# A retention, mixture-of-experts and MLP kernel on one core: a warm-up of 72 small matmuls, tiles amid the turns of attention, and loads in rows of 2 KB

## The reference

```python
# 1. retention: q, k, v are [2, 8, 576, 64]
scores = q @ k.T / 8;  Dmat[h] = gamma_h ** (i - j) for i >= j, else 0
x = ((scores * Dmat) @ v) laid out as [1152, 512]          # tokens x model
# 2. four experts, all used, weighted by p = probs / sum(probs)
out = sum_e p[:, e] * (relu(x @ w1[e]) @ w2[e])            # w1 512x1024, w2 1024x512
# 3. one MLP
h = out @ w_in;  g = h * tanh(softplus(h));  y = g @ w_out # 512x2048, 2048x512
```

## Time and profile before

| | before |
|---|---|
| median of 3 runs | 621.67 us |
| profiled execution, its own time | 622.52 us |
| its span | 620.7 us |
| PE busy / DVE / ACT / POOL | 98% / 43% / 38% / 45% |
| matmuls | 4016 |
| granted PE clock, mean | 0.989 of full |
| DMA | 50.47 MB, mean 81 GB/s |

### The profile page before, as it was taken

The page is one execution under the profiler, slowest core; times in us unless marked ns, Lnnn a source line. Parts: engine busy times, 40 slices in busy tenths (PEclk is TensorE's granted clock), DMA queues, the critical chain, the costliest instruction groups (busy, mean ns, idle before and its releaser), DMA issues.

```text
span 620.7 us, 9829 instructions
## 1 busy us (share of the span) xinstructions
PE 605.9 (98%) x4016; PEld 547.0 (88%) x4016; DVE 264.0 (43%) x361; ACT 234.7 (38%) x434; POOL 278.2 (45%) x230
## 2 busy tenths in 40 slices
PE   6799999999999999999999999999999999999997
PEld 4699799999999999999999999989989999989996
DVE  2467654423154434154534154535545432324334
ACT  2464433322323332223432123435455454334431
POOL 2658645535335544435552535532446553443300
PEclk9699999999999999999999999999999999999999
DMA  8963202332112331112322112321211232201002
GB/s 345 331 213 109 80 35 68 104 101 68 35 35 68 103 103 57 46 35 68 102 84 62 58 34 69 102 69 37 67 34 49 69 105 84 68 1 52 1 1 101
DMA packets 24923, 50.47 MB, mean 81 GB/s; under 512 B 2864, under 2 KB 2992, under 8 KB 24880
## 3 DMA queue, kind: packets, MB, share of 16 engines
q1 hardware_dynamic: 24736, 49.84, 25.1%
q10 hardware_dynamic: 144, 0.02, 0.0%
HBM read 47.49 MB, written 2.36 MB: 80 GB/s over the span
## 4 chain that ended last, share of the span: by engine, by line
PE 92%; DVE 2%; ACT 2%; issue 1%; DMA 1%; POOL 1%; SPq 0%
PE bank L494 30%; PE bank L496 29%; PE bank L495 29%; PE bank L442 1%; DMA loaded<-in_feats 1%; PE bank L470 1%; PE bank L612 1%; PE bank L474 1%; ACT xt L736 0%; ACT w_hi L368 0%; DVE acc_sb L888 0%; DVE acc_sb L892 0%; POOL w_lo L395 0%; DVE xs_a L962 0%; DVE xs_a L959 0%
## 5 line engine op out<-in xcount | busy, mean ns | idle before, releaser
L395 POOL TENSOR_TENSOR w_lo<-w_raw,w_hi 128x512 fp32r<-128x512 f32 x96 | 134.6, 1416 | 149.8 <-ACT w_hi L368 149.8
L494 PE MATMUL bank<-w_hi,h_hi 128*128 128x512 f32 x432 | 168.7, 391 | 0.0
L496 PE MATMUL bank<-w_hi,h_lo 128*128 128x512 f32 x432 | 168.3, 390 | 0.0
L495 PE MATMUL bank<-w_lo,h_hi 128*128 128x512 f32 x432 | 168.3, 390 | 0.0
L875 DVE TENSOR_TENSOR h_act<-part,bank 128x384 f32<-128x384 f32 x96 | 52.9, 551 | 169.9 <-PE bank L496 169.4
L390 POOL TENSOR_TENSOR ws<-ws_f,ws 128x1024 fp32r<-128x1024 f32 x24 | 57.6, 2401 | 145.1 <-ACT ws L364 145.1
L496 PEld LDWEIGHTS bank<-w_hi,h_lo 128*128 128x128 f32 x432 | 81.1, 188 | 16.9
L495 PEld LDWEIGHTS bank<-w_lo,h_hi 128*128 128x128 f32 x432 | 81.1, 188 | 12.3
L494 PEld LDWEIGHTS bank<-w_hi,h_hi 128*128 128x128 f32 x432 | 81.0, 188 | 12.1
L722 ACT ACTIVATE part<-bank 128x384 f32<-128x384 f32 x72 | 35.3, 491 | 138.6 <-PE bank L496 138.6
L842 DVE SCALAR_TENSOR_TENSOR h_lo<-h_act,h_hi 128x384 fp32r<-128x384 f32 x64 | 73.2, 1153 | 20.5 <-ACT h_hi L712 19.9
(11 more groups left out here) (88 smaller groups left out, 863.0 us busy)
## 6 DMA issues: line engine op xcount, KB each, us to landing
w_raw<-in_weights SPq DMA_DIRECT2D x144, 256.0 KB, 2.7
loaded<-in_toks SPq DMA_DIRECT2D x9, 512.0 KB, 7.0
loaded<-in_feats SPq DMA_DIRECT2D x8, 512.0 KB, 6.2
out<-acc_sb SPq DMA_DIRECT2D x6, 256.0 KB, 2.1
out<-acc_sb SPq DMA_DIRECT2D x1, 768.0 KB, 3.5
loaded<-in_first SPq DMA_DIRECT2D x1, 726.0 KB, 4.4
ident<-in_ident SPq DMA_DIRECT2D x1, 64.0 KB, 5.0
p_nat<-in_probs ACTq DMA_DIRECT2D x1, 18.0 KB, 5.1
```

The source lines that it names most:

```text
L395: pool.tensor_tensor(w_lo[layer][:, x], w_raw[:, r % RAW], w_hi[layer][:, x].bitcast(F32), ALU.subtract).then_inc(s_wl, 1)
L494: pe.matmul(out, w[0], x[0], start=first, stop=False, **more)
L495: pe.matmul(out, w[0], x[1], start=False, stop=False, **more)
L496: return pe.matmul(out, w[1], x[0], start=False, stop=last, **more)
```

## The change

- `WARM_START, WARM_NEXT = 7, 5` become `WARM = 72`: 72 zero matmuls of 64x64 weights by 64 columns ahead of the first scores, none behind them.
- Tiles 0, 1, 2, 4 and 5 move from behind `output(c)` to between `scores_and_state(c)` and `output(c)` of the same turn (`TILE_AMID`); 3, 6 and 7 stay behind (`TILE_AFTER`). ACT and DVE take up the tiles amid at the end of their turn.
- The weight jobs of turn 1 and some others move one turn later or join others; `rows(i)` is computed in turns 0 to 3 and not 0 and 4 to 7.
- Features and tokens lie in memory as two blocks of 2 KB rows each, not as one of 4 KB rows; the load has one more dimension, the bytes are the same.
- Behind the turns DVE makes the first two differences before it splits tile 7, and the last `first_lo` comes behind the third and the first `t_lo`; ACT does the two weight jobs before the four `t_hi`.

```diff
-TILES_IN = {3: (0,), 4: (1,), 5: (2, 3), 6: (4,), 7: (5, 6), 8: (7,)}
-JOBS_IN = {1: (("w1", 0, 0),), 2: (("w1", 0, 1), ("w1", 0, 2)), 3: (("w1", 0, 3),), 4: (("w1", 0, 4), ("w1", 0, 5)),
-           5: (("w1", 0, 6),), 6: (("w1", 0, 7), ("w2", 0, 0)), 7: (("w2", 0, 1), ("w2", 0, 2), ("s", 0, 0)),
-           8: (("w2", 0, 3), ("w2", 0, 4)), 9: (("w2", 0, 5),)}
+TILE_AMID = {3: 0, 4: 1, 5: 2, 6: 4, 7: 5}
+TILE_AFTER = {5: 3, 7: 6, 8: 7}
+JOBS_IN = {2: (("w1", 0, 0), ("w1", 0, 1)), 3: (("w1", 0, 2),), 4: (("w1", 0, 3), ("w1", 0, 4)),
+           5: (("w1", 0, 5), ("w1", 0, 6)), 6: (("w1", 0, 7), ("w2", 0, 0)),
+           7: (("w2", 0, 1), ("w2", 0, 2), ("s", 0, 0)), 8: (("w2", 0, 3), ("w2", 0, 4)), 9: (("w2", 0, 5),)}
-ROWS_IN = {4: 5, 5: 6, 6: 7, 7: 8}
+ROWS_IN = {0: (2, 3), 1: (4, 5), 2: (6,), 3: (7, 8)}
-WARM_START, WARM_NEXT = 7, 5
+WARM = 72
...
-                sp.dma_start(slots[:, c % SLOTS, 0:2], feats_in[c - 1]).then_inc(s_feats[c % SLOTS], 16)
+                sp.dma_start(slots[:, c % SLOTS, 0:2].rearrange("p w h c -> p w (h c)"), feats_in[c - 1].rearrange("w p k -> p w k"))\
+                  .then_inc(s_feats[c % SLOTS], 16)
...
-                    pe.matmul(banks[7][:, :], zeros[:, 0:P], zeros[:, :], start=True, stop=True)
+                    pe.matmul(banks[7][HALF[0], 0:CH], zeros[:, 0:CH], zeros[:, 0:CH], start=True, stop=True)
...
-            keep_warm(WARM_START)
+            keep_warm(WARM)
...
-            keep_warm(WARM_NEXT)
             for c in range(PLACES):
                 if has_state(c):
                     scores_and_state(c)
+                if c in TILE_AMID:
+                    early_tile(TILE_AMID[c])
                 output(c)
-                for t in TILES_IN.get(c, ()):
-                    s, i = divmod(t, ITEMS)
-                    plain_ready(s, i)
-                    plain_products(s, i, range(KT))
+                if c in TILE_AFTER:
+                    early_tile(TILE_AFTER[c])
...
+                if c in TILE_AMID:
+                    plain_hi(*divmod(TILE_AMID[c], ITEMS))
+            for job in IN_STAGE[1]:
+                job_hi(act, job)
             for n in range(4):
                 t_hi(0, n)
-            for job in IN_STAGE[1]:
-                job_hi(act, job)
...
-            first_lo(PLACES - 1)
+                if c in TILE_AMID:
+                    plain_lo(*divmod(TILE_AMID[c], ITEMS))
...
+            dve.wait_ge(s_xt, PLACES)
             dve.tensor_tensor(full[0], b12, b11, ALU.subtract).then_inc(s_tf, 1)
-            dve.tensor_tensor(full[2], b22, b12, ALU.subtract).then_inc(s_tf, 1)
             dve.wait_ge(s_tf, 1)
             dve.tensor_tensor(full[1], b22, full[0], ALU.subtract).then_inc(s_tf, 1)
-            dve.wait_ge(s_tf, 3)
+            plain_lo(*divmod(TILE_AFTER[PLACES - 1], ITEMS))
+            dve.tensor_tensor(full[2], b22, b12, ALU.subtract).then_inc(s_tf, 1)
+            t_lo(0, 0)
+            first_lo(PLACES - 1)
+            dve.wait_ge(s_tf, 2)
             dve.tensor_tensor(full[3], full[1], b21, ALU.subtract).then_inc(s_tf, 1)
-            dve.wait_ge(s_tf, 4)
-            for n in range(4):
+            for n in range(1, 4):
                 t_lo(0, n)
```

More of the change, by code:

```diff
@@ L402, in load_feats @@
             def load_feats(c):
-                sp.dma_start(slots[:, c % SLOTS, 0:2], feats_in[c - 1]).then_inc(s_feats[c % SLOTS], 16)
+                sp.dma_start(slots[:, c % SLOTS, 0:2].rearrange("p w h c -> p w (h c)"), feats_in[c - 1].rearrange("w p k -> p w k"))\
+                  .then_inc(s_feats[c % SLOTS], 16)
             def load_toks(c):
-                sp.dma_start(slots[:, c % SLOTS, 2:4], toks_in[c]).then_inc(s_toks[c % SLOTS], 16)
+                sp.dma_start(slots[:, c % SLOTS, 2:4].rearrange("p w h c -> p w (h c)"), toks_in[c].rearrange("w p k -> p w k"))\
+                  .then_inc(s_toks[c % SLOTS], 16)
             def load_weights(r):
@@ L522, in plain_products, with early_tile @@
                     mm.then_inc(s_l1, 1)
+            def early_tile(t):
+                s, i = divmod(t, ITEMS)
+                plain_ready(s, i)
+                plain_products(s, i, range(KT))
             def product(s, j):
@@ L734, in t_hi @@
                 i = T_ORDER[n]
-                act.wait_ge(s_tf, (9, 8, 6, 10)[n] if e else (3, 2, 1, 4)[n])
+                act.wait_ge(s_tf, (9, 8, 6, 10)[n] if e else (2, 3, 1, 4)[n])
                 act.activation(x_sum(i, 0), x_full(e, i), ACT.Copy).then_inc(s_th, 1)
@@ L740, in _ @@
                     first_hi(c - 1)
-                for t in TILES_IN.get(c - 1, ()):
-                    plain_hi(*divmod(t, ITEMS))
+                if c - 1 in TILE_AFTER:
+                    plain_hi(*divmod(TILE_AFTER[c - 1], ITEMS))
                 if has_state(c):
@@ L937, in _ @@
                     masked(c)
-                if c == 0:
-                    for i in range(2, 5):
-                        rows(i)
                 if c > 0:
@@ L946, in _ @@
                     first_lo(c - 1)
[L947 to L950, removed]
+                for i in ROWS_IN.get(c, ()):
+                    rows(i)
+                if c - 1 in TILE_AFTER and c < PLACES:
+                    plain_lo(*divmod(TILE_AFTER[c - 1], ITEMS))
                 if c == PROBS_IN + 1:
                     probs()
-            first_lo(PLACES - 1)
+                if c in TILE_AMID:
+                    plain_lo(*divmod(TILE_AMID[c], ITEMS))
             b11, b21 = xf[:, 0:KH, 0:TC], xf[:, KH:, 0:TC]
@@ L1076 @@
         "first": np.concatenate([tables(), feats[0]], axis=1),
-        "feats": feats[1:],
-        "toks": toks,
+        "feats": feats[1:].reshape(-1, P, 2, KIND).transpose(0, 2, 1, 3),
+        "toks": toks.reshape(PLACES, P, 2, KIND).transpose(0, 2, 1, 3),
         "ident": np.eye(P, dtype=np.float32),
```

## The result

The changed kernel is slower: median 625.5 us of ten runs (623.36 to 627.87), against 621.73 (620.61 to 622.0) for the kernel before on the same chip, ratio 1.006 [1.004, 1.008]. The forecast was 618.4 with a range up to 622.8. The profiled execution took 623.36 (span 621.6), before 622.52 (span 620.7): it is the quickest of the ten, so the trace carries 0.84 us of the 3.8 between the medians, and I come back to the rest.

The account below looks back on a forecast made before the run. It took PE, busy 98%, as the bound, with early holes from fetching 256-instruction pages. Head 4.0 - turns 2.0 + tail 1.3 = 3.3 us less: 618.4 against the median 621.67, range 614.7 to 622.8.

Parts of the forecast that it names:

- I take 5.2: Head: an instruction page takes 5.2 us from asked for to usable, between bounds of 4.4 and 6.0 to 6.3.
- Gain 4.0 us: Head: turn 4 starts at 27.0 us against 31.06, so 4.0 us gained.
- The forecast's own sum with 6.0: Head: with a page turnaround of 6.0 us, turn 4 starts at 29.5, a gain of 1.5 us.
- long with the DMA queues full: Head: page turnaround is 6.0 and 6.3 us at 401 GB/s, shorter (4.8) in a lull at 343.
- The first page: Head: first instruction page asked for at about 5.9 and not 8.2 us, usable at 11.1; 2.3 us of waiting removed once.
- +0.2: Head: PE reaches the first page's boundary at 10.47 + 0.35, when its features land, and waits 0.2 us more.
- Turns 4 to 8 ... loss 2.0 us: Turns 4 and 5: two page boundaries with one-tile turns between lose 1.0 us each; bounds 0.4 and 3.6.
- The same work in another order, 0: Turns 4 to 8: PE is full, so a tile amid a turn has no wait to fill and changes nothing, 0.
- Behind the turns ... Gain 1.3: Behind the turns: the new ACT and DVE order removes the 1.28 us hole ahead of P6; 0 if spare is used up.
- TensorE's clock for tile 0 alone: Head: tile 0's twelve matmuls take 2.2 us, or 3.9 with PE's clock at half.
- rival 3: Warm-up: 72 zero matmuls take 0.107 us each, end at 9.0, first scores 3.8 us late; 623.2 us in all, 13%.
- Rival 1: Head: page turnaround stays 6.0 to 6.3 us; head +1.5, turns 4 and 5 lose, tail +1.3; 621.3 us, 22%.

Follow-up runs that it names:

- e2: The changed kernel with features and tokens loaded in rows of 4 KB as before: 625.23 us, ratio 1.0038 to the kernel before.
- e3: The changed kernel with the order behind the turns as before, on ACT and DVE: 624.66 us, ratio 1.0029 to the kernel before.
- e6: The kernel before with only the warm-up of 72 small zero matmuls: 626.97 us, ratio 1.0085 to the kernel before.
- e9: The changed kernel once more, unedited, in twelve runs: 625.42 us, ratio 1.0036 to the kernel before.
- e10: The changed kernel with ACT's two weight jobs moved behind the copy of P1: 622.02 us, ratio 0.9995 to the kernel before.
- e5: The kernel before with only the new order behind the turns, on ACT and DVE: 621.77 us, ratio 0.9999.
- e7: The kernel before with DVE's new order behind the turns, but ACT's two weight jobs behind the copy of P6: 621.57 us, ratio 0.9992.
- e11: The kernel before with DVE's new order behind the turns and ACT's two weight jobs behind the copy of P1: 621.1 us, ratio 0.9978.
- e12: The kernel before with only the rows of 2 KB: 622.2 us, ratio 1.0004.
- e8: The kernel before without the loads of features and tokens from chunk 4 on, 5.2 MB left out: 618.62 us in one run.
- e4: The kernel before with only tiles amid the turns and the moved weight jobs and rows(): 625.08 us, ratio 1.004.
- e1: The changed kernel with the warm-up of before, 7 + 5 zero matmuls of 512 columns: 626.82 us, ratio 1.0069 to the kernel before.

## Why the prediction was wrong

**The step that failed first: "I take 5.2" for the turnaround, hence "Gain 4.0 us" in the head.** It stayed 6.3: in the changed kernel, boundary at 12.2 (PE starts with features 2 only at 11.75), PE on again at 18.57 and at 24.85, so 6.4 and 6.3. The forecast's own sum with 6.0 gave a gain of 1.5; between the two profiled executions it is 0.56. Neither reason for 5.2 held. The rows of 2 KB were to shorten it, and with rows of 4 KB it is 6.3 as well (e2). The third turnaround of before, 4.8, was taken as a sign of what the change would see. From hole to hole the kernels with 72 zeros (changed, e2, e3, e6, e9, e10) have 6.2 to 6.4 us in seven cases and 5.2 in one (e6); traces with the head of before (before, e5, e7, e11, and e12 but for the rows) have anything from 4.2 to 6.3. The packet shows where the time lies. DMA queues of the changed kernel in the 0.1 us from 16.0 us, where the second such packet starts, form of the earlier trace rows:

```profile
q8 instruction: 1, 0.02, 70.4%
```

It is asked for at about 12.2, starts at 16.0, lasts 1.1, and PE resumes at 18.57: 3.8 us ahead of the packet, 1.1 in it, 1.4 behind it. Only the first differs much between the traces. Stretches from the request (where PE enters a page) to the packet, columns as above, first two of the changed kernel:

```profile
12.20:16.00 3.80, 2.35 (x135) 2.11 (x126) 2.32 (x4) 1.82 (x3) 1.29 (x2) 1.00 1.05 386
18.57:22.40 3.83, 3.48 (x126) 3.34 (x127) 1.25 (x2) 2.18 (x4) 1.33 (x2) 0.62 1.07 391
```

then the third of the kernel before, the second of e11 and the third of e5:

```profile
20.48:22.77 2.29, 2.29 (x109) 2.29 (x112) 1.22 (x2) 0.72 (x2) 2.29 (x3) 0.67 1.01 338
16.04:18.20 2.16, 2.16 (x118) 2.16 (x120) 1.11 (x2) 1.01 (x2) 1.29 (x1) 0.79 1.03 400
21.53:22.50 0.97, 0.97 (x37) 0.97 (x40) 0.00 (x0) 0.00 (x0) 0.97 (x2) 0.50 0.91 348
```

then e8, behind its first hole:

```profile
15.96:17.08 1.12, 1.12 (x72) 1.12 (x76) 0.06 (x1) 0.52 (x1) 0.53 (x1) 0.98 0.10 37
```

At 37 GB/s the packet starts after 1.12 us, at 386 to 391 after 3.8. But the rate doesn't set the wait: at 400 GB/s it is 2.2 us in e11, where the kernel before has 3.7 at 403 (14.20 to 17.9), and 1.0 at 348 in e5 against 2.3 at 338. So "long with the DMA queues full" holds only in part, and why the changed kernel gets the long wait nearly each time stays open. What the runs show is the size: 6.3, where the prediction took 5.2.

**The first page** did come earlier: its packet starts at 9.53 instead of 11.65, and no hole is left at its boundary. The count alone brings it to 10.9 or 11.0 (e2, e6); the rest goes with the rows of 2 KB, which the prediction didn't expect here. But PE starts with features 2 only at 11.75, after 2.03 us of waiting where it had waited for 1.07. One wait took the place of another there; this the prediction had only as "+0.2".

**"Turns 4 to 8 ... loss 2.0 us".** The loss is 1.13, and not where it was put. There is no page hole at the two boundaries in turns 4 and 5; what is left of "issue" is 0.30 at 53.24. The tiles amid separate tiles 2 and 3, and 5 and 6, that stood side by side, so PE changes four times more between 64x64 and 128x128 matmuls. "The same work in another order, 0" was false for this: 0.4 to 0.5 us per pair of changes. That is an estimate from 1.13 less 0.30 over two pairs, and from e3, where the same stretch (30.68 to 56.64) takes 25.96 us with 0.2 of "issue", against 24.91 before. That 72 zeros and tiles amid belong together is shown by the times: e6 alone costs 5.2 us, e4 alone 2.5, both together with the old tail and the rows of 2 KB (e3) 2.1. In the traces each part alone has page holes in turns 4 and 5 (5.3 us and 1.7), both together 0.2.

**"Behind the turns ... Gain 1.3".** P6's hole went, as forecast, and P1, at 64.70, waits for nothing. But the hole moved to P7, and the ledger has -0.3 for both. The prediction looked at P1 and P6 and not at what P7 waits for. The chain of waits of the changed kernel, 10 to 78 us (start us, us, what), tells it:

```profile
68.41 3.47 DVE xt L928 x2
71.87 0.47 DVE h_act L885
72.37 0.53 ACT h_hi L720
72.90 0.39 ACT part L730
```

P7 needs `keep` of P6, which stands on ACT behind `h_hi`, which needs `h_act` on DVE, which stands behind the `t_lo` sums. The change put ACT's jobs ahead of `t_hi`; POOL, released by them, splits five weights in one run, and DVE's sums take 2.05 us instead of 0.95. The last three sums together are 2.7 us longer (1.10, 1.09 and 0.55), and P7 came 2.0 behind its forerunner (71.11 and 0.23 to 73.33). In the kernel before, three of the four sums start beside an idle POOL and take 0.95 to 0.96 us, and the fourth, started 0.3 us after POOL's next split, takes 2.03; ACT is busy beside the first three, so it isn't ACT that slows them. The hole is in e5 too, and it is gone in e10, which differs from the changed kernel by the place of the two jobs alone. No term of the prediction had a price for an engine that slows another.

**The 2.1 us between profiled execution and median.** The prediction priced TensorE's clock for tile 0 alone (2.2 or 3.9 us). (The mean clock of 0.6 of full, told ahead of it for the first slice of 15.5 us, is the second slice's; the first has 0.9.) Four of the ten runs of the changed kernel lie at 623.4 to 623.7 and six at 625.5 to 627.9. e9's trace is of the second kind: half clock behind P7's hole, and half clock for longer in the head. e1's profile has the same behind P7: a hole of 1.8 ahead of it and clock 0.5 from 75.1 to 78.5. In e2 the clock held behind such a hole (1.80), and in e5 (1.66). With the hole away (e10) the median falls by 3.4, of which the traces of the two quick executions explain 1.4 (last matmul 617.99 and 616.57). That the rest is the clock is seen in two profiles and not shown for each run.

**What was right.** The last zero matmul starts at 4.82, and they cost nothing (0.053 us each taken, 3.70 us together measured), so rival 3 falls. The page of 256 instructions and the shift by 120 stand: the holes move into `scores_and_state(2)` and `(3)`. The rows of 2 KB cost nothing in time (e12). Rival 1, "the turnaround stays 6.0 to 6.3", is what the head did; it summed 1.5 - 2.4 + 1.3 = 0.4 us less, where the ledger has 0.56 - 1.13 - 0.3 = 0.9 us more. The rule of the Trainium skill (Runtime: NRT & Kernel Launch, Instruction fetch mechanics) that a crossing is mostly hidden doesn't hold in this head: 6.4 us of "issue" after, 6.7 before. It holds better later: the changed kernel has 0.30 us of "issue" from 30.4 to 56.6. The Trainium skill's rule that a DMA engine changes queue after each packet (DMA: Bandwidth & Descriptors, Queues, rings and completion order) gives half rows under 0.1 us, by the prediction's estimate; the first packet came 1.4 to 1.9 us earlier with them. It doesn't explain 3.8 us ahead of the packet either.

**The sum.** Measured less forecast is 625.5 - 618.4 = 7.1 us. By the ledger the head is 3.4 of it, the order behind the turns 1.6, and the turns cost 0.9 less than forecast. The other 3.0 lie between the profiled executions and the medians: 2.1 above the trace of the changed kernel, and 0.85 by which the profiled execution of before was slower than its median.

**Open.** What the 3.8 us between request and packet consist of, and why that wait is 2.2 us in one trace and 3.7 in another at 400 GB/s. Whether it is the earlier packet or the rows themselves that make features 2 late. The clock's part in the single runs. A middle way, three loads in flight, was not run.

## What to carry to other kernels

Where holes of "issue" come at a fixed pitch of instructions, count where the boundaries fall and what stands ahead of each, as a tile did before where e6 shows a hole; two edits that each move them can cost 5.2 and 2.5 us alone and 2.1 together, so test them together and apart. Read such a stretch in more than one trace before you forecast from it: turn 4 started anywhere from 28.39 to 31.06 with the same head. When you move a job to release another engine sooner, ask what then runs beside the critical engine: a wait removed at one place was given back at the next, since a sum on VectorE took twice its time beside GpSimd. Follow the copy that frees a bank through every engine's list before you book the gain.

## What the runs showed of the hardware

- A 128x768 float32 `tensor_tensor` on DVE took 0.95 us when it started beside an idle POOL (e10, e11) and 2.04 to 2.05 beside POOL's splits of 128x512; the one beside smaller sums on POOL took 1.50. POOL's own sums of 128x256 took 1.46 us beside it and 0.75 with DVE idle.
- Between request and start of a 16 KB packet of instructions lay 1.1 us at 37 GB/s (e8), 1.0 to 2.3 at 338 to 348 (e5, before), and 2.2 to 3.8 at 386 to 403 (e11, before, changed). From the packet's start to PE's going on it was 2.5 to 2.7 us, 1.1 of them the packet itself.
- With 72 zeros ahead, the first such packet started at 9.1 to 9.5 us with rows of 2 KB (changed, e3, e9, e10) and at 10.9 to 11.0 with rows of 4 KB (e2, e6), and PE got features 2 at 11.68 to 12.23 and 10.58 to 10.81. The kernel's time didn't change.
- 72 bf16 matmuls of 128x64 by 64 columns took 3.70 us, 0.051 each.
- TensorE's clock was at half, 1.2 GHz, for 3.4 us behind a hole of 1.8 us in two executions (e9, e1) and at full behind one of 1.8 in two others (the first trace of the changed kernel, e2).
